# Pooled sums of the first pair of heads on TensorE, and an early exponential on ScalarE

## What is computed

```python
q_d = q.reshape(B, H, Sd, factor, D).mean(axis=3)      # factor = 4, Sd = 144; k_d, v_d alike
out_d = sm_attn(q_d, k_d, v_d)                         # softmax(q_d k_d^T / 8) v_d
out_up = np.repeat(out_d, factor, axis=2)
scores = np.where(np.abs(pos[:, None] - pos[None, :]) < factor, scale * q @ k^T, -1e9)
out_local = softmax(scores) @ v
x = out_up + out_local                                 # as (1152, 512)
x = elu(x @ w_in) @ w_out                              # d_ff 2048
out = sum_e p[:, e] * (relu(x @ w1[e]) @ w2[e])        # 4 experts, width 1024
```

## Time and profile before

| | us |
|---|---|
| median of three runs | 640.03 (639.89 to 640.10) |
| the profiled execution | 640.57 |
| its span, first to last instruction | 638.8 |

### The profile page before, as it was taken

The page is one execution under the profiler, slowest core; times in us unless marked ns, Lnnn a source line. Parts: engine busy times, 40 slices in busy tenths (PEclk is TensorE's granted clock), DMA queues, the critical chain, the costliest instruction groups (busy, mean ns, idle before and its releaser), DMA issues.

```text
span 638.8 us, 13097 instructions
## 1 busy us (share of the span) xinstructions
PE 629.7 (99%) x4776; PEld 583.2 (91%) x4776; DVE 350.1 (55%) x765; ACT 284.3 (45%) x786; POOL 322.4 (50%) x278
## 2 busy tenths in 40 slices
PE   8999999999999999999999999999999999999997
PEld 5789999999999999999899899899899889989986
DVE  5866556555668777764354365255265255355352
ACT  4887474756658678443062152152142142242210
POOL 3774545444487999888056065065164163260200
PEclk9999999999999999999999999999999999999999
DMA  9974625142231231221011012011011021010012
GB/s 178 183 216 111 144 67 142 66 106 66 73 126 67 66 129 69 67 67 67 0 67 67 2 66 66 0 66 66 0 66 66 0 68 64 0 67 2 0 50 99
DMA packets 51491, 46.10 MB, mean 72 GB/s; under 512 B 31616, under 2 KB 33920, under 8 KB 51456
## 3 DMA queue, kind: packets, MB, share of 16 engines
q1 hardware_dynamic: 50272, 45.34, 24.5%
q10 hardware_dynamic: 1184, 0.30, 0.2%
HBM read 43.27 MB, written 2.36 MB: 71 GB/s over the span
## 4 chain that ended last, share of the span: by engine, by line
PE 93%; SPq 2%; DVE 2%; ACT 1%; DMA 1%; issue 0%
PE psum L534 16%; PE psum L536 16%; PE psum L535 16%; PE psum L605 11%; PE psum L607 11%; PE psum L609 11%; PE psum L675 2%; PE psum L674 2%; PE psum L673 2%; SPq L329 1%; DMA h_spare<-in_q 1%; PE psum L526 1%; PE psum L519 1%; SPq L314 1%; PE psum L463 1%
## 5 line engine op out<-in xcount | busy, mean ns | idle before, releaser
L1630 POOL TENSOR_TENSOR wb_lo<-wb_raw,wb_hi 128x512 fp32r<-128x512 f32 x64 | 82.0, 1297 | 181.8 <-ACT wb_hi L913 181.6
L1439 DVE SCALAR_TENSOR_TENSOR o_acc<-psum,gate_now,o_acc 128x512 f32<-128x512 f32 x72 | 54.0, 751 | 126.0 <-PE psum L536 125.7
L536 PE MATMUL psum<-wb_hi,h_lo 128*128 128x512 f32 x288 | 112.3, 390 | 0.0
L535 PE MATMUL psum<-wb_lo,h_hi 128*128 128x512 f32 x288 | 112.2, 390 | 0.0
L534 PE MATMUL psum<-wb_hi,h_hi 128*128 128x512 f32 x288 | 112.0, 389 | 0.0
L1021 ACT ACTIVATE h_hi<-psum 128x320 fp32r<-128x320 f32 (+1 forms) x128 | 52.5, 412 | 87.3 <-DVE psum L1411 40.2
L1630 POOL TENSOR_TENSOR wa_lo<-wa_raw,wa_hi 128x512 fp32r<-128x512 f32 x60 | 77.5, 1316 | 16.5 <-ACT wa_hi L952 16.5
L1027 ACT COPY sums<-psum 128x256 f32<-128x256 f32 (+1 forms) x32 | 12.8, 400 | 154.9 <-PE psum L609 154.9
L609 PE MATMUL psum<-x_hi,wa_lo 128*128 128x256 f32 (+2 forms) x228 | 67.4, 296 | 0.0
L605 PE MATMUL psum<-x_hi,wa_hi 128*128 128x256 f32 (+2 forms) x228 | 67.3, 295 | 0.0
L607 PE MATMUL psum<-x_lo,wa_hi 128*128 128x256 f32 (+2 forms) x228 | 67.3, 295 | 0.0
(11 more groups left out here) (193 smaller groups left out, 1663.7 us busy)
## 6 DMA issues: line engine op xcount, KB each, us to landing
wa_raw<-in_moe_w_in SPq DMA_DIRECT2D x8, 1024.0 KB, 5.4
wb_raw<-in_moe_w_out SPq DMA_DIRECT2D x8, 1024.0 KB, 5.1
wa_raw<-in_moe_w SPq DMA_DIRECT2D x8, 1024.0 KB, 5.0
wb_raw<-in_moe_w SPq DMA_DIRECT2D x8, 1024.0 KB, 5.0
out<-o_acc SPq DMA_DIRECT2D x9, 256.0 KB, 2.0
v_win<-in_v SPq DMA_DIRECT2D x20, 80.0 KB, 3.5
q_in<-in_q SPq DMA_DIRECT2D x10, 144.0 KB, 4.3
v_in<-in_v SPq DMA_DIRECT2D x5, 288.0 KB
```

The costliest lines, as they stand in the source:

```text
L535: nc.tensor.matmul(bank_cols, w_hi(n), x_lo_(n), start=False, stop=False)
L536: last = nc.tensor.matmul(bank_cols, w_lo(n), x_hi_(n), start=False, stop=(n == chunks - 1))
L1439: nc.vector.scalar_tensor_tensor(o_acc[:, m, :], psum[:, DOWN2_BANKS[(MT * half + m) % 2], :], gate_now[:, m:m + 1], o_acc[:, m, :], ALU.m ...
L1630: nc.gpsimd.tensor_tensor(lo[:, c, :], raw[:, c, :], hi[:, c, :].bitcast(F32), ALU.subtract).then_inc(lo_ready, 1)
```

## The change

TensorE multiplies each 96x128 tile of q, as weights, by `fours`, a 96x24 matrix that has ones where row p belongs to column p // 4: the result has the features on partitions and the 24 sums of the tile in columns, the same sums that VectorE formed before. They go to PSUM banks 4 (q) and 1 (k), and VectorE copies 144 columns of each. GpSimd builds `fours`. The three fills behind the transposes are gone. ScalarE takes an exponential of a one-column constant first, behind its two loads, and no longer waits for `qTs_ready` ahead of the copy of q.

```diff
-FILL_INPUTS, FILL_SUMS = 9, 3
+FILL_INPUTS = 9
+FIRST_SUM_BANKS = (4, 1)
...
+            def pool_first(tokens_in, loaded, bank):
+
+                pe.wait_ge(loaded[0], 32)
+                for c in range(NLT):
+                    n = LT // FACTOR
+                    last = nc.tensor.matmul(psum[:, bank, n * c:n * (c + 1)], tokens_in[0][:, c, :], fours[:], start=True, stop=True)
+                last.then_inc(first_pooled, 1)
...
             pe.wait_ge(ident_ready, 1)
+            pe.wait_ge(fours_ready, 1)
+            pool_first(q_in, q_loaded, FIRST_SUM_BANKS[0])
             turn_q(0)
+            pool_first(k_in, k_loaded, FIRST_SUM_BANKS[1])
             turn_k(0)
-            fill(FILL_SUMS, 5)
             score(0, 0, ALONE)
...
                 act.wait_ge(q_turned, u + 1)
-                if isinstance(u, int) and u == 0:
-                    act.wait_ge(qTs_ready, 1)
-
...
                 act.dma_start(k_in[0][:, :, HD * h:HD * (h + 1)], k_pairs[0][:, :, h, :]).then_inc(k_loaded[0], 16)
+            act.wait_ge(exp_input_set, 1)
+            nc.scalar.activation(first_exp[:, 1:2], first_exp[:, 0:1], ACT.Exp).then_inc(first_exp_done, 1)
             copy_qT(0, ALONE)
...
-            def take_first_sums(first, turned, sums_, ready):
-
-                dve.wait_ge(turned, 1)
-                nc.vector.tensor_reduce(sums_[0][:, 0:POOLED].rearrange("p (a j) -> p a j", a=2),
-                                        psum[:, first:first + 2, 0:HALF].rearrange("p a (j r) -> p a j r", r=FACTOR), X, ALU.add
-                                        ).then_inc(ready, 1)
+            def take_first_sums(n, sums_, ready):
+
+                dve.wait_ge(first_pooled, n + 1)
+                nc.vector.tensor_copy(sums_[0][:, 0:POOLED], psum[:, FIRST_SUM_BANKS[n], 0:POOLED]).then_inc(ready, 1)
...
             nc.vector.memset(zeros[:], 0.0).then_inc(zeros_set, 1)
+            nc.vector.memset(first_exp[:, 0:1], 0.0).then_inc(exp_input_set, 1)
...
             pool.wait_ge(const_step, 6)
             pool.sem_inc(band_ready, 1)
+            nc.gpsimd.memset(fours[:], 1.0).then_inc(const_step, 1)
+            for step, sign in enumerate((1, -1)):
+                pool.wait_ge(const_step, 7 + step)
+                nc.gpsimd.affine_select(out=fours[:], in_=fours[:], compare_op=ALU.is_ge, fill=0.0,
+                                        base=step * (FACTOR - 1), pattern=[[-sign * FACTOR, LT // FACTOR]],
+                                        channel_multiplier=sign).then_inc(const_step, 1)
+            pool.wait_ge(const_step, 9)
+            pool.sem_inc(fours_ready, 1)
```

More of the change, by code:

```diff
@@ L189, in program @@
         zeros = sb1("zeros", [128, 512], BF16)
+        fours = sb1("fours", [LT, LT // FACTOR])
+        first_exp = sb1("first_exp", [128, 2])
         attention_only.close()
@@ L246, in program @@
         const_step, ident_ready, band_ready = sem("const_step"), sem("ident_ready"), sem("band_ready")
+        fours_ready, first_pooled, exp_input_set, first_exp_done = sem("fours_ready"), sem("first_pooled"), sem("exp_input_set"), sem("first_exp_done")
         zeros_set, pad_set, acc_zeroed = sem("zeros_set"), sem("pad_set"), sem("acc_zeroed")
@@ L1481, in _ @@
             dve.wait_ge(pad_set, 3)
-            take_first_sums(IN_BANKS[ALONE][0], q_turned, qTs, qTs_ready)
-            take_first_sums(IN_BANKS[ALONE][1], k_turned, kTs, kTs_ready)
+            take_first_sums(0, qTs, qTs_ready)
+            take_first_sums(1, kTs, kTs_ready)
             take_kT(0)
```

## The result

| | before | changed |
|---|---|---|
| median of nine runs, us | 640.10 (639.89 to 640.58) | 642.18 (642.02 to 645.89) |
| ratio | | 1.0052, 95% interval 1.0040 to 1.0064 |
| the profiled execution, us | 640.57 | 645.76 |
| its span, us | 638.8 | 644.0 |

What follows compares the result with a forecast made beforehand. The opening was taken as bound by SyncE's loads up to the fourth q's landing; the path shift of +0.05 us vanished in its 0.47 us gap, so no change: 640.0 us, range 639.4 to 640.9.

Steps and rivals of the forecast that it cites:

- The second rival: Opening: without the profiler the fourth q lands 0.5 us earlier, so the computing path's gain counts fully; 639.5 us, chance 0.08.
- without slack: From the fourth q's transposes to the first projection, 18 us run engine to engine, passing on any delay outlasting the gap.
- The price of a pooled record: Time of one trace record of the q and k matmuls with `fours`: taken as 63 ns, bounds 37 and 92.
- P: Time of one group of 12 records of matmuls with `fours`, for q or k: 0.76 us at 63 ns a record.
- the break-even of 0.97: Group time in us, 81 ns a record, above which the opening's delay outlasts the 0.47 us gap at the fourth q.
- T0: Start of the zeroing matmul ahead of the first scores: 7.36 us before, forecast 7.61 at 63 ns a record.
- d: Shift of the computing path at pair 0, (T0 - 7.36) - 0.20: +0.05 us at 63 ns a record.
- the rival of dear weight loads: TensorE's matmuls with `fours` cost 81 ns or more a record, so the delay outlasts the gap; 640.3 to 641.5 us, chance 0.12.
- the low end: The 37 ns bound for a record, where copying the sums of k was said to delay the first scores to 7.05.
- The clock: Rival: without the fills and with 24-column matmuls, TensorE returns to 1.2 GHz until the fourth q lands; about 645 us, chance 0.03.
- The 0.20 us behind T0: Path behind the first scores' start, shorter by this because local scores no longer wait for the copy of q.
- The rival of a second table load ahead of the first exponential: ScalarE loads its table again before the first real exponential, 1.28 us on pair 0's path; 640.9 us, chance 0.01.

Runs made afterwards that it cites:

- no_sum_fills: The kernel before without its three fills behind the transposes, nothing else changed: 640.50 us, ratio 1.0003 to before.
- exp_alone: The kernel before plus only the early exponential of a constant, the copy of q still waiting for `qTs_ready`: 639.74 us, ratio 0.9987 to before.
- pool_alone: The changed kernel without its early exponential: 643.63 us, ratio 1.0053 to before; its profile is of a run at 642.60 us.
- turns_first_96: The changed kernel with both transpose groups ahead of both pooled groups and `fours` 96 columns wide: 641.84 us, ratio 1.0024 to before.
- fills_12: The changed kernel with 12 fills ahead instead of 9: 641.35 us, ratio 1.0020 to before; its profile is of a slower run, 642.90 us.
- fours_96: The changed kernel with `fours` 96 columns wide instead of 24, same weight loads: 641.32 us, ratio 1.0016 to before.
- the slow group: Runs of the unaltered changed kernel near 645.8 us, three of its nine timed runs (645.69 to 645.89) and its profiled execution.
- turns_first: The changed kernel with both transpose groups ahead of both pooled groups, `fours` still 24 columns wide: 643.59 us, ratio 1.0049 to before.
- q3_early: The kernel before with the fourth q's load issued ahead of the four window loads of v of pair 1: 640.41 us, ratio 1.0003 to before.

## Why the prediction was wrong

**What bounds the opening: one execution taken for the rule.** I took the landing of the fourth q at 20.74 for a hold that gives back nothing of a gain and covers a loss up to 0.47 us. The row was true of one execution. In the traces of no_sum_fills and exp_alone the same transposes start 0.45 and 0.58 us earlier and wait for nothing, moving that load shows no gain, and exp_alone is faster at the end. The second rival, the early gain arrives, had this right and got 0.08. A hint was in the trace: SyncE's second issue of that load took 1.87 us in it, for 1.22 in exp_alone and 1.05 in the changed kernel, and I took one landing time for a steady one.

That nothing covers a delay is not shown either, as the way behind those transposes is not "without slack". From them to the first projection it is 18.4 us in the profile of before and 18.7 in no_sum_fills, but 17.8 in eight of the nine profiles of kernels with pooled sums (18.2 in pool_alone), which all get there later. In turns_first_96 the zeroing matmul stands 3.01 us later than before (10.37 for 7.36) and the first projection 1.46 us, a part of which is its other order.

**The price of a pooled record: mis-sized.** I took 63 ns and called 92 the ceiling, as six loads of the same tile pass in 0.55 us in the transposes. At 2.4 GHz it is 105 ns (fills_12) and 107 ns (pool_alone, (8.60 - 7.31)/12), so P = 1.26 us and over the break-even of 0.97. The bound carried over from the transposes did not hold for the matmuls that are no transposes. The rule that I set aside, the Trainium skill's "TensorE: Matmul & The Clock Gate", section "LDWEIGHTS (loading the stationary operand)", gives 107 ns for 128 columns. At 2.4 GHz these traces agree with it; at 1.2 GHz a record takes 212 ns. With P = 1.26 my own sum gives T0 = 8.61 and d = 1.05, which is 640.6 us with 0.47 covered and 641.1 with nothing covered. So the price alone, put into the sum as I made it, would have left the time within my range. The kernels in which the level mostly held were at 641.3 (fours_96, ratio 1.0016) and, with three more fills, 641.0 in the faster group of fills_12. So the rival of dear weight loads, which had 0.12, names some 0.8 of the 2.1 us that the median lost, with the interval of fours_96 reaching from 0.4 to 1.6. (The 7.05 for T0 at the low end does not follow from its terms either, which give 6.97; nothing hangs on it.)

**The clock: the step that failed.** The mechanism was among the rivals, with 0.03. I argued that TensorE would have no idle time between 4.99 and T0, and that 0.45 us of it had brought no drop. Both were true and neither bears on it: 1.13 us of idle time brought no drop in the profile of no_sum_fills, and in fills_12 and pool_alone the level fell with no idle time ahead of the fall. The time I gave for it, 645, is near the slow group. That is partly luck: the low level lasted to 16.6 us there, not to the landing of the fourth q, and the groups themselves cost more than I took. The rest of the loss, 1.2 us of the median and 4.8 in the slow group, is 1.2 GHz over a part of the opening, and turns_first against turns_first_96 shows that the 24 moving columns bring it. Which group a run falls in, with the same instructions, varies from run to run, as does the moment at which the level first rises: ahead of the transposes at 4.99 in the profile of before, but within those of k, from 6.12 to 6.85, in that of q3_early, where those of q still take 0.99 us. I have not shown what decides it.

**What held.** The table load near 2 us, the copies of 0.31 us, GpSimd's `fours` ahead of its use, the sum of v at 10.6, and qT copied long before the local scores (at 9.72, for 14.19). The 0.20 us behind T0 were of the right sign and a little low in exp_alone: the second row maximum stands 1.84 us behind the zeroing matmul, for 2.12, and 0.2 us of it is left at the fourth q. In the profile of the changed kernel they drown in the low clock, where the row maximum stands 3.01 us behind.

The rival of a second table load ahead of the first exponential (0.01) did not come: there is none in the opening.

## What to carry to other kernels

Work moved onto TensorE costs its weight loads when few columns move, here 105 ns for each record of 24 columns, and it can cost the clock besides: look at the distances between matmuls ahead of and behind such a group, in more than one execution. A one-element activation in idle time puts a table load where it costs nothing; that half of the change alone is worth 0.7 us here (0.3 to 1.4 by its interval), and is the version to keep. A wait that is the last by some tenths of a microsecond in one profile is no bound: read a second execution before a gain is written off against it.

## What the runs showed of the hardware

- A record of an f32 matmul with a 96x128 tile as weights takes 105 ns at 2.4 GHz (fills_12) and 212 ns at 1.2 GHz (the changed kernel) with 24 columns moving, and 112 ns at 2.4 GHz with 96 (turns_first_96). A transpose of the same tile takes 92 and 165 ns.
- TensorE fell from 2.4 to 1.2 GHz while it was busy without a gap, in or right behind the groups with 24 columns (fills_12, pool_alone), and held its level through 1.13 us of idle time (no_sum_fills).
- The granted clock reads 1.00 over the fills in the profiles of the kernel before, the changed kernel, fills_12 and pool_alone, though the fills run at 1.2 GHz there; the slow group of the changed kernel, which stays at that level to 16.6 us, has a mean granted clock of 1.000, and its faster group 0.997. In these traces the distances tell the level in the opening, and the column does so only once it has changed.
